# Attention on one core: the last 64 tokens of a pair first, two value matmuls in place of three

## The reference

```python
scores = scale * np.matmul(q, k.transpose(0, 1, 3, 2))
thresh = np.max(scores, axis=-1, keepdims=True) - tau
scores = np.where(scores >= thresh, scores, -1e9)
attn = np.exp(scores - np.max(scores, axis=-1, keepdims=True))
attn = attn / (np.sum(attn, axis=-1, keepdims=True) + 1e-09)
return np.matmul(attn, v)
```

## Time and profile before

| | us |
|---|---|
| median of three runs | 940.68 |
| profiled execution, its own time | 929.86 |
| its span, first to last instruction | 928.1 |
| TensorE busy in the span | 822.7 |
| VectorE busy | 456.2 |
| ScalarE busy | 401.9 |
| POOL busy | 505.2 |
| attention stage (last copy of its last rows ends) | 327.25 |

### The profile page before, as it was taken

The page is one execution under the profiler, slowest core; times in us unless marked ns, Lnnn a source line. Parts: engine busy times, 40 slices in busy tenths (PEclk is TensorE's granted clock), DMA queues, the critical chain, the costliest instruction groups (busy, mean ns, idle before and its releaser), DMA issues. The chain is left out here.

```text
span 928.1 us, 17386 instructions
## 1 busy us (share of the span) xinstructions
PE 822.7 (89%) x5424; PEld 697.4 (75%) x5425; DVE 456.2 (49%) x1046; ACT 401.9 (43%) x672; POOL 505.2 (54%) x455
## 2 busy tenths in 40 slices
PE   2989999999998823899999999998475999999998
PEld 1778888888877612688888888886345999999898
DVE  3867787877777263122212211221473665546622
ACT  2667777877777540112211212221554544434400
POOL 3556665665698703946698878950655431503200
PEclk9899999999999965899999999999787999999999
DMA  9976577667647054485655445561310110110001
GB/s 225 326 172 163 145 171 185 153 154 177 174 113 195 13 194 151 145 270 170 226 181 181 169 159 181 183 217 44 107 35 17 35 57 25 35 57 1 33 20 52
DMA packets 81441, 123.17 MB, mean 133 GB/s; under 512 B 28352, under 2 KB 41920, under 8 KB 81408
## 3 DMA queue, kind: packets, MB, share of 16 engines
q1 hardware_dynamic: 71280, 99.34, 37.0%
q0 software_dynamic: 3472, 11.28, 4.1%
q10 hardware_dynamic: 6656, 12.13, 3.9%
HBM read 70.55 MB, written 23.86 MB: 102 GB/s over the span
## 5 line engine op out<-in xcount | busy, mean ns | idle before, releaser
L320 POOL TENSOR_SCALAR p_ring<-p_ring,rsum 128x576 f32<-128x576 f32 x144 | 107.2, 752 | 93.3 <-DVE rsum L409 93.1
L459 PE MATMUL psum<-k_st,q_st 128*128 128x288 f32 x640 | 124.9, 323 | 26.4 <-DMA q_st<-q_split 17.2
L376 DVE TENSOR_REDUCE negmax<-psum 128x1 f32<-128x576 f32 x144 | 108.2, 752 | 73.2 <-PE psum L459 72.0
L459 PEld LDWEIGHTS psum<-k_st,q_st 128*128 128x128 f32 x640 | 94.1, 198 | 39.3 <-issue 26.8
L959 PE MATMUL psum<-w_split,x_hi 128*128 x352 | 118.7, 408 | 1.7 <-DVE x_lo L1039 1.7
L391 DVE SCALAR_TENSOR_TENSOR p_ring<-psum,thresh,e_ring 128x576 f32<-128x576 f32 x144 | 116.7, 810 | 6.0 <-PE psum L476 3.2
L980 PE MATMUL psum<-w_split,h_hi 128*128 x352 | 115.4, 399 | 3.2 <-DVE h_lo L1044 3.2
L902 POOL TENSOR_TENSOR w_split<-w_raw,w_split 128x1024 fp32r<-128x1024 f32 x48 | 115.0, 2396 | 4.0
L514 ACT ACTIVATE e_ring<-psum,negmax 128x576 f32<-128x576 f32 x144 | 107.7, 748 | 19.2 <-DVE negmax L376 16.3
L546 ACT COPY p_t<-psum 128x512 f32<-128x512 f32 (+1 forms) x192 | 107.7, 561 | 16.9 <-PE psum L472 13.1
L1308 PE MATMUL psum<-tok_hi,z_hi 128*128 128x288 f32 x288 | 87.6, 304 | 10.7 <-DVE z_lo L1211 10.7
(11 more groups left out here) (184 smaller groups left out, 1569.6 us busy)
## 6 DMA issues: line engine op xcount, KB each, us to landing
w_raw<-w_dram SPq DMA_DIRECT2D x48, 512.0 KB, 3.4
k_st<-k_split SPq DMA_DIRECT2D x64, 288.0 KB, 5.0
q_st<-q_split SPq DMA_DIRECT2D x60, 144.0 KB, 2.5
xs_dram<-stage SPq DMA_DIRECT2D x23, 256.0 KB, 2.0
xs_nat<-xs_dram ACTq DMA_DIRECT2D x22, 256.0 KB, 3.0
ys_dram<-y_nat ACTq DMA_DIRECT2D x22, 256.0 KB, 2.2
k_nat<-k_t_dram SPq DMA_DIRECT2D x16, 288.0 KB, 4.4
q_nat<-q_t_dram SPq DMA_DIRECT2D x16, 288.0 KB, 4.6
```

The lines of the kernel that those rows point to most:

```text
L320: pl.tensor_scalar(t, t, rsum[:, k % BODY:k % BODY + 1], 1.0, ALU.mult, ALU.mult).then_inc(s_norm, 1)
L376: dve.tensor_reduce(negmax[:, k % 3, 0:1], s_bank[k % 3][:, :, 0:HALF], AX.XY, ALU.max, negate=True).then_inc(s_max, 1)
L459: mm = pe.matmul(bank[:, x, 0:HALF], lhs, key[:, HALF * x:HALF * x + HALF], start=(j == 0), stop=(j == len(terms) - 1))
```

## The change

The tile of both heads' last 64 queries becomes the first of a pair (u = 0) and the eight full tiles follow. The transposed probabilities `p_t[0]` get room for 320 columns: the first four full tiles' 256 and those 64. The value product is then two groups, of 320 and of 256 columns, and the third group goes: 16 groups a pair, not 17. The steps of the groups are now: step 0 "t", then "pv" 1 of the pair before, then "k" 2 (now of the new pair's own first tile); step 1 "t" and "r" 1 of the pair before (three row matmuls); step 4 "k" 0; step 5 "pv" 0; step 6 "r" 0 (two row matmuls); step 8 "k" 1. What a group waits for is now written into the table (`need`): the group before the last one, or the one that it reads.

On ScalarE, where a step holds a value group, the exponentials of the next step are computed ahead of the copy of that group. On VectorE, for tiles 3 and 7 of a pair (`alone`), the mask of tile k stands ahead of the maximum of tile k+1, and the threshold of k+1 moves into the next step, behind the maximum of k+2.

The small arrays (`sums`, `rsum`, `negmax`, `thresh`) move to the end of a buffer that the expert layer uses later, since `p_t[0]` takes more room; the zeroing of the end of `x_t` goes, and ScalarE waits for five zeroings, not seven. The row matmuls read `x_t` at the columns 0, 128 and 320, 448, 256; the last of them has 64 real queries and 64 that nothing reads.

```diff
-    p_t = [sb(f"p_t{a}", [P, 2, KT, 2 * P], F32) for a in range(2)]
+    COLS = (2 * P + REM, 2 * P)
+    p_t = [sb(f"p_t{a}", [P, 2, KT, COLS[a]], F32) for a in range(2)]
...
-        before = {0: [("pv", 2, m - 1)], 1: [("r", 0, m - 1)], 2: [("r", 1, m - 1)]}.get(u, []) if k >= LEAD else []
-        after = {3: [("k", 0, m)], 4: [("pv", 0, m)], 7: [("k", 1, m)], 8: [("pv", 1, m), ("k", 2, m)]}.get(u, [])
-        return before + here + after
+        before = {0: [("pv", 1, m - 1)], 1: [("r", 1, m - 1)]}.get(u, []) if k >= LEAD else []
+        after = {0: [("k", 2, m)] if here else [], 4: [("k", 0, m)], 5: [("pv", 0, m)], 6: [("r", 0, m)],
+                 8: [("k", 1, m)]}.get(u, [])
+        return here + before + after
...
-            if k >= TILES and k % TILES in (0, 1, 4, 5):
+            if k >= TILES and k % TILES in (1, 2, 5, 6):
...
+        def alone(k):
+            return k % TILES in (3, 7)
+
         def step(i, k, first=False, last=False):
             ends = (k - 1) % BATCH_OF == BATCH_OF - 1 and not (first and k < 1)
-            if not (last and k + 1 >= BODY):
+            follows = not (last and k + 1 >= BODY)
+            swap = alone(k) and not (first and k < TILES // 2)
+            if follows and not swap:
                 row_max(i, k + 1)
+            if alone(k - 1) and not (first and k - 1 < TILES // 2):
+                row_thresh(i, k)
             if ends:
                 sum_eps(i, k - 1)
             if not (last and k >= BODY):
                 mask(i, k)
             if ends:
                 recip(i, k - 1)
-            if not (last and k + 1 >= BODY):
-                row_thresh(i, k + 1)
+            if follows:
+                if swap:
+                    row_max(i, k + 1)
+                else:
+                    row_thresh(i, k + 1)
...
-            if u < TILES - 1:
-                h, at = u % 2, P * (u // 2) + (u % 2) * (S + 2 * REM)
+            if u > 0:
+                h = (u - 1) % 2
+                at = P * ((u - 1) // 2) + h * (S + 2 * REM)
                 parts = [(q_st[m][:, at:at + P], h)]
...
-            if not (isinstance(i, int) and i == 0 and n < 2):
-
-                pe.wait_ge(s_free, PER_ITER * i + n - (0 if (what, arg) == ("pv", 2) else 1))
+            if not (isinstance(i, int) and i == 0 and need < 1):
+                pe.wait_ge(s_free, PER_ITER * i + need)
...
-                n = REM if arg == 2 else 2 * P
                 for t in range(KT):
                     for h in range(2):
-                        mm = pe.matmul(bank[D * h:D * h + D, 0:n], v_sb[m % 2][:, h, t, :], p_t[arg % 2][:, h, t, 0:n],
+                        mm = pe.matmul(bank[D * h:D * h + D, 0:COLS[arg]], v_sb[m % 2][:, h, t, :], p_t[arg][:, h, t, :],
                                        start=(t == 0), stop=(t == KT - 1))
...
         def step(i, k, groups, last=False):
-            if not (last and k + AHEAD_E >= BODY):
-                exp(i, k + AHEAD_E)
-            for n, what, arg, m in groups[k]:
+            def ahead(k):
+                if not (last and k + AHEAD_E >= BODY):
+                    exp(i, k + AHEAD_E)
+
+            if not values(k - 1, groups):
+                ahead(k)
+            for n, what, arg, m, _ in groups[k]:
+                if what == "pv":
+                    ahead(k + 1)
                 group(i, n, what, arg, m, k)
```

More of the change, by code:

```diff
@@ L143, in groups_of_step @@
         here = [("t", u, m)] if not (last and k >= BODY) else []
[L144 to L146 removed]
+        before = {0: [("pv", 1, m - 1)], 1: [("r", 1, m - 1)]}.get(u, []) if k >= LEAD else []
+        after = {0: [("k", 2, m)] if here else [], 4: [("k", 0, m)], 5: [("pv", 0, m)], 6: [("r", 0, m)],
+                 8: [("k", 1, m)]}.get(u, [])
+        return here + before + after
+    SOURCE = {("pv", 0): ("k", 0), ("pv", 1): ("k", 1), ("r", 0): ("pv", 0), ("r", 1): ("pv", 1)}
     def numbered(first, ks, last=False):
[L150 removed]
+        table, at = {}, {}
         for k in ks:
             table[k] = []
[L153 to L154 removed]
+            for what, arg, m in groups_of_step(k, last):
+                need = first - 1
+                if (what, arg) in SOURCE:
+                    need = max(need, at[SOURCE[what, arg] + (m,)] + 1)
+                table[k].append((first, what, arg, m, need))
+                at[what, arg, m] = first
                 first += 1
@@ L163, in attention @@
     assert PER_ITER % 2 == 0
-    KEYS_DONE = {(arg, m): n + 1 for k in LOOP for n, what, arg, m in LOOP[k] if what == "k"}
-    V_DONE = [next(n for k in LOOP for n, what, arg, m in LOOP[k] if (what, arg, m) == ("pv", 2, mm)) + 1 for mm in range(2)]
-    ROWS_DONE = [next(n for k in LOOP for n, what, arg, m in LOOP[k] if (what, arg, m) == ("r", 1, mm)) + 1 for mm in range(2)]
+    KEYS_DONE = {(g[2], g[3]): g[0] + 1 for k in LOOP for g in LOOP[k] if g[1] == "k"}
+    V_DONE = [next(g[0] for k in LOOP for g in LOOP[k] if g[1:4] == ("pv", 1, mm)) + 1 for mm in range(2)]
+    ROWS_DONE = [next(g[0] for k in LOOP for g in LOOP[k] if g[1:4] == ("r", 1, mm)) + 1 for mm in range(2)]
     def sync(sp):
@@ L486, in group @@
                 rhs = turn[:, bass.ds((2 * i + m) % DC, 1), :].rearrange("p o n -> p (o n)")
-                for j, t in enumerate(range(3) if arg == 0 else range(3, KT)):
-                    mm = pe.matmul(bank[:, j * W:(j + 1) * W], x_t[m][:, t * P:t * P + P], rhs, start=True, stop=True)
+                for j, at in enumerate(ROW_COLS[arg]):
+                    mm = pe.matmul(bank[:, j * W:(j + 1) * W], x_t[m][:, at:at + P], rhs, start=True, stop=True)
             mm.then_inc(s_filled, 1)
@@ L497, in step @@
                 scores(i, k + AHEAD_S)
-            for n, what, arg, m in groups[k]:
-                group(i, n, what, arg, m, k)
+            for n, what, arg, m, need in groups[k]:
+                group(i, n, what, arg, m, need, k)
         pe.wait_ge(s_ident, 16)
@@ L520, in group @@
             act.wait_ge(s_filled, PER_ITER * i + n + 1)
-            if what == "t" and u < TILES - 1:
-                c, h = u // 2, u % 2
+            if what == "t" and u > 0:
+                c, h = (u - 1) // 2, (u - 1) % 2
                 dst = p_t[c // 2][:, h, 0:FULL, c % 2 * P:c % 2 * P + P]
```

40 lines of the change are left out of this document (21 added, 19 removed).

## The result

| | before | after |
|---|---|---|
| median, us | 937.67 (20 runs, 934.46 to 941.51) | 940.62 (20 runs, 937.79 to 943.01) |
| last copy of the last rows of attention ends, us | 327.25 | 330.15 |
| mean period, from pair 3's start to pair 13's (ten periods) | 18.03 | 18.26 |

What follows compares the result with a forecast made beforehand. TensorE was taken to pace attention at 18.03 us a pair, the key chain hidden by 0.4 us; +0.3+0.56+1.6-0.2+0.3 = +2.6 us on 940.68 gave 943.3, range 935 to 950 (forecast's own 940.7 to 946).

Steps and rivals of the forecast that it cites:

- pairs 2 and 3: Early attention pairs, waiting for k_st: a later start shows partly in pair 2, +0.3 us, and wholly in pair 3, +0.56.
- the ten regular pairs: Pairs 4 to 13 of attention: ten periods, each 0.16 us longer on average, together +1.6 us.
- the tail: End of attention, from pair 15: weights come 0.9 us earlier, last value group and copies end 1.2 later, +0.3 us.
- the key chain taking over from TensorE: First tile's scores through POOL's split to k_st copies: grows 0.56 us against 0.3 and 0.5 slack, making the period 18.2.
- pairs 14, 15: Attention pairs paced by POOL, which also splits weights: -0.2 us, since its wait for the next sums goes.
- I take 0.13, nearer to the upper end: VectorE, threshold between first tile's maximum and the mask: costs between 0.04 and 0.2 us, taken as 0.13.
- TensorE alone gains about 0.25 us a pair: 17.8: TensorE's own work per pair: one mask stall goes, a similar one comes behind the double tile, period 17.8 us.
- The cause is the order on ScalarE: TensorE's mask stall, nearer to 0.4 us: exponentials wait behind the value product's copy, which has waited 1.31 us for TensorE.
- copies and groups one after the other: Last value groups and copies in the tail, run in sequence: 13.1 us to the end, 11.9 before, so +1.2.
- Rival A: First tile's chain grows by less than its slack, so TensorE's saving counts: about -2.4 us, 938.3; chance 0.15.
- Rival B: TensorE's mask stall and small waits near copies also go, 0.85 us less a pair: 932.2; chance 0.10.
- Rival C: Last k_st copy lands 6.9 us after issue, not 5.4 to 5.6, +1.4 a pair: some 957; chance 0.13.

Runs made afterwards that it cites:

- early keys: Changed kernel, but POOL splits q low, k high and k low right behind q high, ahead of the normalisation that waits for the old pair's sums: period 17.99 us.
- before_keys_slower: Kernel before with one more 128x576 pass on POOL, its result unread, ahead of the last key split: period 18.27 us.
- two_groups_last_keys: Changed kernel with the double tile last, 320 columns in the second value group, threshold at once, keys split early: period 18.06 us.

## Why the prediction was right or wrong, point by point

The forecast was +2.6 us. The ratio says +2.5, and attention's end +2.90. That agreement is luck: of the five terms two have the wrong sign (pairs 2 and 3, +0.86 forecast, -1.39 measured) and two are too small (the ten regular pairs by 0.66, the tail by 1.87), and they cancel. The mechanism, the key chain taking over from TensorE, was right; what was mis-sized in it is the threshold, taken at 0.13 us and measured at 0.25.

| term | predicted | measured | from |
|---|---|---|---|
| pair 2 | +0.3 | -0.64 | start 51.94, was 52.58 |
| pair 3 | +0.56 | -0.75 | period 18.30, was 19.05 |
| pairs 4 to 13 | +1.6 | +2.26 | 252.84 - 70.24 = 182.60, was 180.34 |
| pairs 14, 15 | -0.2 | -0.14 | 36.73, was 36.87 |
| tail from pair 15's start | +0.3 | +2.17 | 40.58, was 38.41 |
| sum | +2.6 | +2.90 | |

*The base.* The absolute 943.3 took the median of three runs, 940.68, as the kernel's time. Over 20 runs it is 937.67. The measured 940.62 is 2.7 below the forecast, and the base alone was 3.0 too high: three runs that spread over 4 us don't fix a median to tenths of a per cent. The forecast's own range has a slip too: its upper bounds (0.6, 0.63, 2.3, -0.2, 1.2) add up to +4.5, 945.2, not 946.

*The key chain takes over: held, and shown.* The early keys (18.26 to 17.99) and the slowed keys (0.40 of slack) are one experiment from each side. Scores to maximum 1.36 (predicted 1.34), maximum to threshold 0.67 (0.68), mask to maximum 0.81 (0.80), maximum to mask 0.73 (0.74), mask to normalisation 1.11 (1.12). The step that failed is "I take 0.13, nearer to the upper end": from threshold to mask it is 0.25 (108.89 to 109.14), above even the upper bound of 0.2. The row taken for the lower end had an instruction behind the threshold that doesn't read it; none of the earlier trace rows had a mask directly behind its own threshold. Over the pairs the head grew by 0.64, from 4.29 in the mean, against a mean slack of 0.41 (0.63 from landing to start, less the 0.22 of a true wait). That makes 0.23 a period where 0.56 and 0.40 had made 0.16, and 0.226 is measured; ten times 0.07 is what this term of the sum missed.

*"TensorE alone gains about 0.25 us a pair: 17.8": failed.* With the threshold where the change puts it, TensorE alone needs 17.99; with the threshold at once, 17.63. That a stall would come back two tiles behind the double tile was right (110.02); its size was not. From the start of the transposes ahead of them to those scores it is 1.04, where without a wait it is 0.36, so 0.68 are lost; the old stall was 0.4. The threshold's late place makes the difference: 0.36 of TensorE's time, 0.25 in the chain.

*"The cause is the order on ScalarE": not borne out.* The old orders with the early keys give 17.65, the new ones 17.63. In this layout the two orders, taken together, bring a regular pair nothing. Whether they were it in the kernel before, where a third group stood behind the first tiles, no run here tells.

*Pairs 2 and 3: wrong sign.* Pair 2:

```profile
51.94 1.33 PE L482 MATMUL psum<-k_st,q_st 128*128 128x288 f32 x8 [1.72 <-DMA k_st<-k_split]
...
70.24 1.32 PE L482 MATMUL psum<-k_st,q_st 128*128 128x288 f32 x8
```

It waits 1.72 us for k_st, not 3.11. For pair 3 the copies are issued at the same time as before (last at 64.5) and land 5.5 later, where it was 6.9:

```profile
L213 SPq DMA_DIRECT2D k_st<-k_split x2: 822/1154/1485, 63.7 to 64.5; - x2
...
DMA to landing us min/median/max: 5.0/5.3/5.5
```

The prediction let the chain grow and kept the landing. The landing fell by 1.4 instead, in this kernel as in every other with two value groups whose keys are not early (5.4 to 5.6 us, also with the double tile last). Why it fell is open. The store of x stands 2 us earlier in SP's queue here, at 52.28 and not 54.43; it starts at 52.0 to 53.1 in all of those kernels, and at 56.03 in before_keys_slower, where the landing takes 6.9 again. The two go together; moving the store alone was not tried.

*Pairs 14 and 15: the number held, -0.14 for -0.2, the reason only in part.* Pair 15 starts 18.55 behind pair 14, 18.83 before (-0.28). But pair 14 starts 18.18 behind pair 13, 18.03 before, and 0.22 behind its keys' landing: it is still paced by the key chain, and grows like the regular pairs.

*The tail: failed by its size.* The weights come earlier, as predicted:

```profile
290.82 2.15 SPq L42 DMA_DIRECT2D stage<-w_dram  x4
...
295.42 1.05 POOL L53 TENSOR_SCALAR w_split<-stage 128x1024 fp32r<-128x1024 f32 x1 [0.27 <-DMA stage<-w_dram]
```

POOL stands 0.27 for them, not 2.29, and lets TensorE go 314.71 - 289.57 = 25.14 after the pair's start, 26.55 before: -1.41 (predicted -0.9). From there it takes 15.44, where it took 11.86: +3.6 (predicted +1.2, 13.1 us in all). The step that failed is "copies and groups one after the other", priced at full clock. At full clock it takes 13.12, as the run with the moved weight piece shows, close to the 13.1 of the sum; the 2.3 us above that are the lower clock behind TensorE's stall of 3.54 us, which the prediction left out.

*Rival A, the copy in time:* not in this kernel. The early keys make it so, and the ratio then is 0.9997, 0.3 us less than before, where A had 2.4 less: TensorE alone was not 17.8. *Rival B, TensorE's stalls go as well:* "it needs the key copies earlier than now" was its condition; it needed the early threshold too. With both, 931.55 against 938.07, 6.5 us (5.9 by the ratio); B had forecast 8.5 less. *Rival C, later landings:* didn't occur. Landings stayed at 7.4 to 7.6 us behind the split's end in all regular pairs.

*The signs.* The period near 18.2, the head (4.9 for 4.8) and the group of 2.9 us came. "Waits of L459 for the DMA of k_st in nearly every pair" didn't show as such lines, save for pairs 2 and 15: the wait is there, by the landing, but covered by the modelled end of the row matmuls. Nor did the waits for the mask go (0.44 at 110.02).

*The weight loads as a measure.* The rule of the Trainium skill (Perfetto Trace Analysis, Identifying the Most-Contended Engine) left nearly a fifth of TensorE unused. The best period found is 17.63; there the loads are busy 31.75 of 40 us:

```profile
100.00:140.00 40.00, 39.65 (x311) 31.75 (x310) 32.87 (x97) 31.42 (x58) 24.68 (x33) 1.00 0.64 164
```

That is 79%, 78% in the changed kernel and 81% before, though the period differs by 0.6 us and the work by a group. Of the fifth a ninth was to be had by these edits (18.03 to 17.63, 2.2%). What it needs beyond that, no run here shows.

## What to carry to other kernels

Before work is taken off an engine that looks full, measure the slack of the chains that run beside it: for a copy, its landing against the first instruction that needs it, less what that distance is where the engine truly waits; a saving beyond the slack buys nothing until the chain is shortened too. A small instruction whose result the very next one on its engine reads cost 0.25 us here though it lasts 0.14, and nothing that could be seen where another stood between, so that is where it belongs. When a sum of terms comes out right, compare it term by term before it is believed, and take the base from more runs than three. The end of a stage in one execution can carry a microsecond that no edit made; compare the stretches that an edit touches.

## What the runs showed that I had not expected

- Threshold to the mask that reads it: 0.25 us from start to start on VectorE, for an instruction of 0.14 us. With the threshold ahead of that maximum, and so another instruction between, the mask started 0.67 behind the maximum, as if the threshold weren't there.
- Behind a stall TensorE ran at a lower granted clock for some microseconds: after 3.54 us of standing, 0.59 for 7.1 us (320 columns in 4.36 and not 2.91). The length of the stall alone doesn't say when: behind 1.78 us (the run with the moved weight piece) a 256-column group took 4.03, behind 1.88 us at 315.39 in the kernel before it took 2.38. Ahead of pair 2 the clock fell behind 2.12 us in one execution (0.66 over the next 5 us), and stayed full behind 3.38 us in another (two_groups_last_keys). What tells these apart was not tried.
- From the landing of the last copy to the first matmul that waits for it: 0.22 to 0.27 us in every such pair of every kernel, mostly 0.22 or 0.23.
- A wait of 0.27 us can be absent from the view of waits, since the modelled ends of the matmuls ahead of it reach over it.
